# Gate weights on one Trainium2 core: only Strassen sums made anew, plain tiles stored from SBUF, second superblock in opposite order

## The reference

```python
# attention: q, k, v are (4, 8, 576, 64)
out_d = sm_attn(mean4(q), mean4(k), mean4(v))        # 144 positions, repeated 4 times
local = softmax(scale * q @ k.T where |i-j| < 4) @ v # banded
x = (repeat(out_d, 4) + local)  -> (2304, 512)
# first MLP, gated: w1, w2 (512, 1024), w3 (1024, 1024), w_out (1024, 512)
y = (((x @ w1) * (x @ w2)) @ w3) @ w_out
# second MLP: u1, u2, u3 (512, 768), u_out (768, 512)
out = max(y @ u1, y @ u2, y @ u3) @ u_out            # float32
```

## Time and profile before

| | us |
|---|---|
| runs of before | 717.03, 718.29, 721.27 (median 718.29) |
| the profiled execution | 715.15 |
| its span, first to last instruction | 713.4 |
| PE busy in it | 681.4 (96%) |
| DVE, ACT, POOL busy | 400.2, 275.4, 366.8 |
| mean DMA share of 16 engines (q1) | 74.4% |

### The profile page before, as it was taken

One profiled execution on the slowest core, in us unless ns is written; L12 is line 12 of the kernel. 1 busy time (PEld: TensorE's weight loads), 2 busy tenths in 40 slices (PEclk: granted clock), 3 DMA queues, 4 the chain that ended last, 5 costly groups with the idle time before them and its releaser, 6 DMA issues.

```text
span 713.4 us, 16907 instructions
## 1 busy us (share of the span) xinstructions
PE 681.4 (96%) x6848; PEld 648.3 (91%) x6848; DVE 400.2 (56%) x755; ACT 275.4 (39%) x590; POOL 366.8 (51%) x368
## 2 busy tenths in 40 slices
PE   8999999998979999999799897999999999999998
PEld 7878989987869899999789897999999999999997
DVE  4465555444466553447434364457775677746673
ACT  5465344434434334456444364022241222412221
POOL 6989578967875234446145335024382243813441
PEclk9999999999979999999999999999999999999999
DMA  9884477777775869987999667996669766697632
GB/s 306 268 276 139 138 213 222 209 223 218 229 232 155 247 204 293 342 294 260 317 360 315 231 227 277 416 359 226 229 235 401 243 227 222 247 409 248 210 141 88
DMA packets 97820, 180.04 MB, mean 252 GB/s; under 512 B 7760, under 2 KB 47952, under 8 KB 96976
## 3 DMA queue, kind: packets, MB, share of 16 engines
q1 hardware_dynamic: 97744, 178.98, 74.4%
HBM read 137.53 MB, written 41.42 MB: 251 GB/s over the span
## 4 chain that ended last, share of the span: by engine, by line
PE 72%; DMA 13%; SPq 4%; DVE 4%; issue 3%; POOL 2%; ACT 2%; ACTq 0%; DVEq 0%; POOLq 0%
PE psum L824 23%; PE psum L825 21%; PE psum L826 21%; DMA gate_weights_stream<-room 6%; DMA attention<-wb 4%; PE psum L863 2%; DMA weights_stream<-attention 2%; PE psum L841 2%; PE psum L834 1%; PE psum L872 1%; PE psum L851 1%; DMA attention<-ident 1%; SPq L741 1%; ACT attention L1392 1%; DMA attention<-qk 1%
## 5 line engine op out<-in xcount | busy, mean ns | idle before, releaser
L1616 POOL TENSOR_TENSOR second_split<-xy,second_split 128x384 fp32r<-128x384 f32 x99 | 104.6, 1075 | 164.5 <-ACT second_split L1392 164.5
L824 PE MATMUL psum<-second_split,weights_split 128*128 128x384 f32 x402 | 135.7, 338 | 0.8 <-DVE sums L1298 0.6
L826 PE MATMUL psum<-second_split,weights_split 128*128 128x384 f32 x402 | 134.9, 336 | 0.0
L825 PE MATMUL psum<-second_split,weights_split 128*128 128x384 f32 x402 | 134.9, 336 | 0.0
L824 PE MATMUL psum<-weights_split 128*128 128x384 f32 x278 | 94.7, 341 | 12.3 <-DMA weights_split<-weights_stream 4.2
L826 PE MATMUL psum<-weights_split 128*128 128x384 f32 x278 | 93.2, 335 | 0.0
L825 PE MATMUL psum<-weights_split 128*128 128x384 f32 x278 | 93.0, 334 | 0.0
L1616 POOL TENSOR_TENSOR weights_split<-xy,weights_split 128x384 fp32r<-128x384 f32 (+1 forms) x65 | 74.3, 1160 | 23.7 <-ACT weights_split L1392 23.4
L824 PEld LDWEIGHTS psum<-second_split,weights_split 128*128 128x128 f32 x402 | 76.0, 189 | 2.6 <-DVE sums L1298 1.5
L825 PEld LDWEIGHTS psum<-second_split,weights_split 128*128 128x128 f32 x402 | 76.0, 189 | 0.0
L826 PEld LDWEIGHTS psum<-second_split,weights_split 128*128 128x128 f32 x402 | 75.9, 189 | 0.0
(11 more groups left out here) (143 smaller groups left out, 1453.8 us busy)
## 6 DMA issues: line engine op xcount, KB each, us to landing
weights_split<-weights_stream SPq DMA_DIRECT2D x39, 768.0 KB, 5.3
weights_split<-gate_weights_stream SPq DMA_DIRECT2D x112, 256.0 KB, 4.7
weights_split<-weights_stream SPq DMA_DIRECT2D x54, 512.0 KB, 5.9
weights_stream<-attention SPq DMA_DIRECT2D x48, 256.0 KB, 3.2
xy<-wa SPq DMA_DIRECT2D x40, 256.0 KB, 5.5
attention<-qk SPq DMA_DIRECT2D x16, 576.0 KB, 4.6
weights_stream<-attention SPq DMA_DIRECT2D x24, 384.0 KB, 3.4
gate_weights_stream<-room SPq DMA_DIRECT2D x16, 448.0 KB, 5.4
```

The source lines that it names most:

```text
L824: pe.matmul(out, lhs[:, 0], rhs[:, 0], start=first, stop=False, skip_group_check=read_between)
L825: pe.matmul(out, lhs[:, 0], rhs[:, 1], start=False, stop=False, skip_group_check=read_between)
L826: return pe.matmul(out, lhs[:, 1], rhs[:, 0], start=False, stop=last, skip_group_check=read_between)
L1616: return pool.tensor_tensor(out, full, high.bitcast(F32), ALU.subtract)
```

## The change

- **Gate preparations.** Of a preparation only the four sums are made: POOL's four additions write four new slots (`gsum_b`) instead of working in the eight-slot buffer; the copy on ACT and the low part on POOL cover 512 columns instead of 1024; two stores of 256 KB instead of three (256, 192, 448 KB). The buffers are three deep; a raw load waits for the additions of n-3 (`gs_made`) instead of for stores to land (`gmade_out`), and POOL's additions wait for the stores of n-3. The three plain tiles of each block are stored from the split w1 and w2 in SBUF (`store_tiles`, 24 steps of two DMAs of 128 KB, at positions 70 to 139).
- **Second streamed superblock in opposite order.** It takes the weight blocks 7 to 0 (`weights_of`), so the seven operands of block 7 stay in their places (`place_plan`) and 105 loads remain of 112. Its last layer sums over f in the order 6, 7, 4, 5, 2, 3, 0, 1 (`F_ORDER`). Its first results have buffers of their own.
- **Preparations for the second MLP.** 11 instead of 12 stand ahead of the second streamed superblock, then 5, then 8 instead of 7. The raw load of n stands at 10 units ahead of its `copy_raw`, or 2.7 units behind that of n-3, instead of at 4.5 ahead. `high_wb` and `low_wb` stand 0.6 and 0.9 units later.
- **First ring groups.** The loads of the first four groups wait only for the first four preparations' stores and stand at 25, 19, 13 and 7 units ahead of B_BEGIN. The twelfth `split_y` (steps 11 to 13 write to other memory now) waits for the end of the last layer instead of for all stores.

```diff
+FIRST_READY, FIRST_GROUPS = 4, 4
+STREAMED = (6, 5, 7, 3, 1, 2, 4)
+GSUMS = 4
+F_ORDER = [list(range(F1)), [f for fp in range(GP) for f in (F1 - 2 - 2 * fp, F1 - 1 - 2 * fp)]]
...
-    return [PROLOGUE + 4 + 4.6 * n + late for n in range(GPREPS)]
+    return [PROLOGUE + 3.5 + 4.6 * n + late for n in range(GPREPS)]
...
-    at = [25, 36, 46] + [58 + 3.3 * n for n in range(9)] + [91 + 11 * n for n in range(5)] + [147 + 3.3 * n for n in range(7)]
+    at = [26, 36, 46] + [57 + 3.6 * n for n in range(8)] + [93 + 10.5 * n for n in range(5)] + [146 + 3.3 * n for n in range(8)]
...
+    return [(max(G_BEGIN + 20.5 + n, at[n] - 10, at[n - RAWS] + 2.7 if n >= RAWS else 0), ("RAW", n)) for n in range(PREPS)]
...
             def load_gate_raw(n):
-                if n >= GMADE:
-                    sp.wait_ge(gmade_out[(n - GMADE) % 2], GMADE_INC * ((n - GMADE) // 2 + 1))
...
+                ge(sp, gs_made, n - GMADE + 1)
+                sp.dma_start(graw_b[n % GMADE], wc[n].rearrange("p (e c) -> p e c", e=GSUMS)).then_inc(wc_in[n % GMADE], 16)
...
+            def store_tiles(u, e):
+
+                f, w = 2 * (u // 2) + (e == 4), u % 2
+                sp.wait_ge(w12_lo, 2 * f + w + 1)
+                own = w12[:, :, f, w, (0 if e == 1 else 1):KD:2, :].bitcast(F32)
+                to = product_dram(u, e).rearrange("p (k s c) -> p s k c", k=KP, s=2)
+                for i in range(2):
+                    sp.dma_start(to[:, i], own[:, i]).then_inc(tiles_out, 16)
...
+            def load_first_group(i):
+                for n in range(FIRST_READY - 2, FIRST_READY):
+                    sp.wait_ge(*stored(n))
+                load_group(i)
...
-                                 [(max(at, PROLOGUE + 1), ("GATE_RAW", n)) for n, at in enumerate(gate_preparations(-4.5))],
-                                 [(at, ("GATE_OUT", n)) for n, at in enumerate(gate_preparations(8.4))],
...
+                                 [(max(at, PROLOGUE - 1), ("GATE_RAW", n)) for n, at in enumerate(gate_preparations(-5))],
+                                 [(at, ("GATE_OUT", n)) for n, at in enumerate(gate_preparations(7))],
+                                 [(PROLOGUE + 6 + 3 * (3 * u + i), ("GATE_TILES", u, e)) for u in range(GUNITS) for i, e in enumerate((1, 2, 4))],
+                                 raw_loads(), [(B_BEGIN - 25 + 6 * i, ("GROUP", i)) for i in range(FIRST_GROUPS)],
...
                 elif Y_SPLIT[(e, kp)] == 11 and s == 0:
 
-                    for i in range(2):
-                        act.wait_ge(made_out[i], 3 * 16 * PREPS // 2)
+                    act.wait_ge(last_done, 2 * JO * GATED)
...
             def combine_wc(n):
 
-                made = gmade_b[n % GMADE]
+                raw, made = graw_b[n % GMADE], gsum_b[n % GMADE]
                 pool.wait_ge(wc_in[n % GMADE], 16 * (n // GMADE + 1))
...
+                ge(pool, gmade_out[n % GMADE], 32 * (n // GMADE))
```

178 lines of the change are left out of this document (104 added, 74 removed).

## The result

The changed kernel takes **687.84 us** in the median (686.58 to 688.68); the kernel before took 717.66 us (713.59 to 721.27) beside it. The ratio is 0.9585, 95% interval 0.953 to 0.9639.

A forecast was written before the change was run, and what follows sets the result against it. PE's waits (some 22 us) and lower clock (6 us) were taken as what could be gained. Attention stretch 12.0, second streamed superblock 7.1 and second MLP's start 2.0 make 21.1 us: 718.3 to 697.2 us, range 689 to 710.

The forecast's parts named there:

- The upper bounds of the prediction: Whole kernel: all gains at their upper bounds, 8.1 + 0.6 + 6.3 + 7.6 + 5.9 = 28.5 us, hence 689.8 us.
- The late load of q and k: Attention stretch: without SP's wait for landed stores the load follows the scores, and waits for `x_out` shrink; gain 7.7 us.
- The cover of 4.7 us: Attention stretch: the load of q and k may be issued up to 4.7 us behind the scores at no cost.
- The sign that I had set: Attention stretch: PE's scores wait for `x_out` under 1 us in all.
- POOL: Attention stretch: POOL has 17.4 us less work, but only the 0.6 us that PE waited for it is gained.
- The clock: Attention stretch: 3.7 us of lower-clock time goes with the waits of 2.4 and 3.3 us; bounds 0 and 6.3.
- Second streamed superblock: Earlier raw loads and one preparation fewer ahead remove PE's waits behind ACT; gain 7.1 of 7.6 us.
- Border: Start of the second MLP: the ring's 4.2 us wait goes, a 2.2 us wait for ACT comes; gain 2.0 us.
- The 9.1 us worked out for a ring group: Second MLP: the fifth group arrives 9.1 us after PE's end, needed at 11.6 us, so it costs 0.
- From the profiled time to the median: Whole kernel: the median of 718.29 us, 3.1 us above the profiled execution, was the base for the forecast.
- The first rival: Attention stretch: SP stays late, waiting for POOL's low parts and the tiles; 12.0 us stay lost, 709.2 us; chance 0.13.
- the second (a free border, 693.3 us): Start of the second MLP: ACT catches up or `split_y` does not block; 2.2 + 1.7 us more gained; chance 0.12.

The follow-up runs named there:

- the second trace of the changed kernel: The changed kernel run once more with no edit; median 687.18 us, its profiled execution 690.64 us.
- the fastest kernel: Changed kernel with three `split_y` behind `gated_y` on ACT, one DVE scaling ahead of `make_x`, and ACT's last gate-sum copy behind the copy for `x_out`: 682.4 us.
- the small stores: Changed kernel with 48 additional stores of 8 KB on SP beside those of the split tiles: 690.31 us, ratio 0.9677.

## Why the prediction was right in kind and too high in size

In short: the places and what ended last there were right. The time came out below the range by the last step, from the profiled execution to the median (2.7 us), and by gains that the sum had put too low: the clock (2.5 us), the second streamed superblock (2.2 us) and the first (1.3 us). The upper bounds of the prediction, 28.5 us in all, covered the 27.7 us of the trace; they did not cover the change of that last step.

**The late load of q and k: right.** The issue came 0.04 us behind the scores, SP's waiting was gone, and putting back its one wait cost 11.8 us. The cover of 4.7 us was not too large either: 4.7 us late cost `x_out` nothing, 6.7 and 8.8 us late cost it. But the size came out by some luck. From start to start of the same matmuls, the four visits S gained 6.7 us (forecast 7.7) and V 0.7 (0.6). The sum, 8.0 us with all that is new against a forecast of 8.3, is near because a wait put down to "issue", at 238.7 us, fell by 1.1 us, which I had not counted, while PE lost 0.5 us ahead of 140 us. The first is at least in part scatter: the second trace of the changed kernel has such a wait of 0.7 us at that place. The sign that I had set, waits for `x_out` under 1 us in all, was missed: they were 1.5.

**POOL: the step failed, without harm to the sum.** I wrote that POOL's relief was worth 0.6 us and "nothing more, since the rest of POOL is off PE's path". That was read from a trace in which SP was last at every S. With SP early, POOL is next: 11.7 us of load put back on it cost 5 us, 23.4 us cost 10. For what is late next I had left 0.2 us at each of two visits; it was 1.5 us at one visit.

**The clock: mis-sized.** I took 3.7 us in the attention stretch, and left the 0.6 us behind T's wait and the 1.7 at the border as lost. Where no wait stands in either trace, the lead of the changed kernel grows only by the clock. It grows by 1.2 us from 165 us of the kernel before on (forecast 1.6), by 2.1 from 201 on (2.1), by 1.6 behind T's wait (0) and by 1.3 at the border (0): 6.2 us instead of 3.7. A stretch of 5 us had also shown only a part of T's loss; the next one has more of it:

```profile
215.00:220.00 5.00, 5.00 (x119) 4.51 (x119) 3.21 (x4) 1.78 (x4) 2.99 (x4) 0.87 0.12 42
```

But the 1.6 and 1.3 us are luck of the profiled execution: T's wait was still 2.0 us, the border's 2.2, and the second trace of the changed kernel lost 3.4 us behind just these two. So what I left as lost is lost in some executions only; the 3.1 us between the two traces are as large as half of the trace's part of the miss.

**First streamed superblock: left out.** It gained 1.3 us where I had no term. Three short waits of the kernel before, at 285.8, 297.6 and 299.1 us, make 0.9 of it.

**Second streamed superblock: mis-sized by 2.2 us.** I took 7.1 of 7.6 us; it was 9.3. Half of this is how idle time is shown. Rows of PE in the changed kernel, ahead of the border's wait:

```profile
416.84 0.33 PE L895 MATMUL psum<-weights_split 128*128 128x384 f32 x1
...
417.01 0.34 PE L896 MATMUL psum<-weights_split 128*128 128x384 f32 x1
...
419.56 0.44 PE L894 MATMUL psum<-second_split,weights_split 128*128 128x384 f32 x1 [2.21 <-ACT xy L1463]
```

A matmul is shown for 0.34 us, but the next one starts 0.17 us behind it when nothing is in the way. So PE lost 419.56 - 417.01 - 0.17 = 2.38 us where the row says 2.21. Each wait is longer than its row by some 0.17 us. In this stretch the gaps (the six of the earlier trace rows, and one too short to be listed) make 8.7 us from start to start, against 7.6 in the earlier trace rows. The 0.5 us that I kept back for small waits did not come, and the last 0.6 us of the 9.3 I can't place. As for the cause, the first wait was the backlog of preparations, as I said; that the late raw loads explain the others needs the close preparations beside them.

**Border: right to 0.1 us in its wait.** The chain that I added up from single durations (3.3 us on ACT, less 1.04) is there row by row, and PE waits 2.2 us:

```profile
417.01 0.92 ACT L1463 ACTIVATE attention<-psum 128x896 fp32r<-128x896 f32 x1
...
417.82 0.51 ACT L1463 ACTIVATE second_split<-xy 128x384 fp32r<-128x384 f32 x1
...
418.24 0.48 ACT L1463 ACTIVATE xy<-psum 128x384 f32<-128x384 f32 x1
...
418.61 0.52 ACT L1463 ACTIVATE second_split<-xy 128x384 fp32r<-128x384 f32 x1
...
419.02 0.49 ACT L1463 ACTIVATE xy<-psum 128x384 f32<-128x384 f32 x1
```

The 9.1 us worked out for a ring group whose `high_wb` stands behind the twelfth `split_y` showed itself as a wait of 9.5 us, when the first groups were loaded late.

**From the profiled time to the median: failed.** The 3.1 us between them were carried over as if they were a constant. But they were scatter: executions of the kernel before lie between 709.35 and 721.49 us, with clock losses from 7.1 to 15.7 us, and the profiled one happened to be below their median. The changed kernel's executions lie within 4.3 us, and the offset was 0.4 us. A forecast for the profiled execution would have been 694.0 against 687.46.

**Rivals and the page's rule.** The first rival's 709 us was far off, and the second (a free border, 693.3 us) was nearest, though by the clock and not by its own mechanism, as the wait was there in full. The page "DMA: Bandwidth & Descriptors" of the Trainium skill, sections "Rules for kernel authors" and "Anatomy of one DMA", would have had 32 more DMAs of 128 KB cost 64 us, an estimate for the case that nothing overlaps. Its 2.0 us stand there for a DMA that GpSimd issues; here SyncE issues them all, which the prediction did not say. The change had the 32 DMAs and gained 29.8 us. The profile's list of DMA issues of the changed kernel has the stores with the median time from issue to landing:

```profile
gate_weights_stream<-weights_split SPq DMA_DIRECT2D x48, 128.0 KB, 3.6
```

They land 3.6 us behind their issue, beside PE's work. 48 more on top cost 10 to 11 us, not 96 by the same estimate. So with the DMA engines at 0.81 of their time the runs show no cost, and at 0.98 they show one in the rule's direction, by another way: SP gets to the load of q and k too late.

## What to carry to other kernels

Put no wait for a landing ahead of a load that others need in the same queue: let it wait for the reader of the old data, and check how late the next load may be, since inside that cover 4.7 us cost nothing here. When the last arrival at a wait is removed, size the next one by giving it load, not from the old trace, where it has slack that it owes to the first. And treat the difference between a profiled execution and a median as scatter, not as a term.

## What the runs showed of the hardware

The clock falls from its upper level (2.4 GHz) to its lower (1.2 GHz) behind waits of PE of some 2 us in some executions and not in others, at the same place and in the same code: behind T's wait of 2.0 us the mean clock over 200 to 210 us is 1.00 in one trace of the changed kernel and 0.83 in the other. Two falls made that trace 3.1 us longer. Waits of up to 1.3 us were followed by no fall in any of the four executions of the fastest kernel; behind one of 1.7 us, at 91.5 us, the changed kernel's clock stayed up, and with the stores doubled it fell.

In three kernels that bring waits back, the clock costs as much as the waits or more. The clock loss is 7.0 to 13.4 us with SP's old wait, 5.6 to 8.4 with two additions on POOL and 5.6 to 7.0 with the stores doubled, against 0 to 3.4 in the changed kernel.

An issue on SP's queue has no fixed length. For the load of q and k it takes 0.33 to 0.35 us in all twelve cases of the changed kernel in which SP was idle before it (0.33 at 178.94 us). Right behind another issue it takes 0.39 to 0.55 us there, 0.62 us in the earlier trace rows, 0.61 at 175.08 us with the stores doubled, and in single cases up to 1.5 us (at 134.03 us with the small stores). So a list of back-to-back issues costs more than a lone issue suggests: the 48 additional stores are 35.3 us of SP when full and 30.1 us when they are 8 KB, 0.74 and 0.63 us each.
